# Banded attention in front of two expert layers: the order of q/k loads and x stores on SyncE, and the step in which the next pair is transposed

## The reference, cut to what matters

```python
def _attn_ref(q, k, v, n_global, n_local):          # q, k, v: (4, 8, 768, 64)
    scores = matmul(q, k.T) / sqrt(D)
    keep = is_global | is_local                      # key < 8, or 0 <= row - key < 96
    scores = where(keep, scores + bias, -1e9)        # bias = -slope[head] * distance
    a = exp(scores - max);  a = a / (sum(a) + 1e-9)
    return matmul(a, v)

x = attn.transpose(0, 2, 1, 3).reshape(3072, 512)
x = _moe_ref(x, ...)       # 8 experts, each token to its best one; 512 -> 1024 -> 512
return _moe2_ref(x, ...)   # 8 experts, 384 tokens each, assigned by falling logit
```

## Time and profile before

| | |
|---|---|
| time, median of 3 runs | 1249.87 us (1248.23 to 1251.53) |
| profiled execution: its own time / span | 1250.35 us / 1248.7 us |
| attention, first scores to last product with v | 14.35 to 324.8 us of the span |
| PE busy over the span | 982.6 us (79%) |
| DVE busy over the span | 760.6 us (61%) |
| ACT busy over the span | 411.6 us (33%) |
| queue of SP's transfers | 99.67 MB, 26.7% of 16 engines' span |

### The profile page before, as it was taken

The page is one execution under the profiler, slowest core; times in us unless marked ns, Lnnn a source line. Parts: engine busy times, 40 slices in busy tenths (PEclk is TensorE's granted clock), DMA queues, the critical chain, the costliest instruction groups (busy, mean ns, idle before and its releaser), DMA issues.

```text
span 1248.7 us, 22576 instructions
## 1 busy us (share of the span) xinstructions
PE 982.6 (79%) x6264; PEld 836.7 (67%) x6265; DVE 760.6 (61%) x1994; ACT 411.6 (33%) x885; POOL 193.8 (16%) x242
## 2 busy tenths in 40 slices
PE   7867787878835999999999995122227999999995
PEld 4656666667734788888888884121217889999884
DVE  5656565656675668878786877555564445544441
ACT  3434343434451543442453441000002334433320
POOL 2121111211000111112111111100002122233310
PEclk8888787878976999999999997555556999999998
DMA  8343443434410615343432413000001444455300
GB/s 191 88 98 93 90 97 86 100 82 97 163 68 26 232 35 177 111 157 116 169 119 101 171 70 108 19 1 0 0 0 51 152 168 146 158 184 185 118 26 26
DMA packets 146021, 127.31 MB, mean 102 GB/s; under 512 B 102381, under 2 KB 114669, under 8 KB 145840
## 3 DMA queue, kind: packets, MB, share of 16 engines
q1 hardware_dynamic: 137168, 99.67, 26.7%
q0 software_dynamic: 8800, 27.01, 6.3%
HBM read 107.78 MB, written 20.71 MB: 103 GB/s over the span
## 4 chain that ended last, share of the span: by engine, by line
PE 47%; DVE 15%; issue 6%; DVEq 3%; ACT 1%; ACTq 1%; DMA 0%; POOL 0%; POOLq 0%
PE ps_o L1150 9%; PE ps_s L1127 8%; PE ps_o L1519 7%; PE ps_s L1503 6%; PE ps_pT L1503 5%; DVE product L1348 4%; PE ps_s L1519 4%; PE ps_t L1677 2%; PE ps_pT L1138 1%; PE ps_t L960 1%; DVEq L1351 1%; DVE arena_t L1768 1%; DVE w_split_parts L1339 1%; PE ps_t L1490 1%; PE ps_t L1113 1%
## 5 line engine op out<-in xcount | busy, mean ns | idle before, releaser
L1150 PE MATMUL ps_o<-w_split_parts,hs 128*128 x696 | 170.4, 401 | 9.9 <-ACT hs L1226 9.1
L1127 PE MATMUL ps_s<-w_split_parts,xs 128*128 x696 | 167.9, 397 | 2.3 <-issue 1.4
L1150 PEld LDWEIGHTS ps_o<-w_split_parts,hs 128*128 128x128 f32 x696 | 131.4, 192 | 38.5 <-issue 11.3
L1348 DVE SCALAR_TENSOR_TENSOR product<-y_sb,wg_all 128x512 bf16<-128x512 f32 x232 | 151.0, 689 | 7.2 <-ACT y_sb L1244 2.2
L1127 PEld LDWEIGHTS ps_s<-w_split_parts,xs 128*128 128x128 f32 x696 | 130.1, 190 | 29.6 <-issue 3.4
L638 DVE CUSTOM_DVE_ANT_0 arena_p<-ps_s,arena_b 128x256 f32<-128x256 f32 (+1 forms) x144 | 54.1, 392 | 113.9 <-PE ps_s L442 57.0
L758 ACT ACTIVATE arena_p<-arena_p,min_s 128x256 f32<-128x256 f32 (+1 forms) x192 | 91.8, 484 | 12.0 <-DVE min_s L638 10.6
L1519 PE MATMUL ps_o<-w_split_parts,hs 128*128 128x512 f32 x384 | 94.2, 397 | 0.0
L1339 DVE TENSOR_TENSOR w_split_parts<-raw,w_split_parts 128x1024 f32 (+1 forms) x68 | 78.7, 1221 | 5.7 <-ACT w_split_parts L1237 4.4
L1546 ACT ACTIVATE xs<-ps_t 128x512 fp32r<-128x512 f32 x22 | 13.2, 600 | 206.2 <-PE ps_t L1490 206.1
L1519 PEld LDWEIGHTS ps_o<-w_split_parts,hs 128*128 128x128 f32 x384 | 70.2, 188 | 16.1 <-ACT hs L1553 2.9
(11 more groups left out here) (287 smaller groups left out, 1842.3 us busy)
## 6 DMA issues: line engine op xcount, KB each, us to landing
raw<-in_moe_w SPq DMA_DIRECT2D x32, 2048.0 KB, 9.4
y_rows<-y_sb POOLq DMA_DIRECT2D x31, 256.0 KB, 2.3
kn<-in_k SPq DMA_DIRECT2D x32, 192.0 KB, 3.4
qn<-in_q SPq DMA_DIRECT2D x32, 192.0 KB, 3.5
vn<-in_v SPq DMA_DIRECT2D x32, 192.0 KB, 2.8
x_rows<-arena_x SPq DMA_DIRECT2D x96, 64.0 KB, 1.6
va<-in_v SPq DMA_DIRECT2D x32, 120.0 KB, 2.6
wg_rows<-in_moe_w_gate SPq DMA_DIRECT2D x1, 2048.0 KB, 7.6
```

Source lines behind the costliest of these rows:

```text
L1127: last = nc.tensor.matmul(ps_s[:, f, :], xs[:, a, c * P:(c + 1) * P], weights(par, w, cols), start=(n == 0), stop=(n == len(passes) - 1))
L1150: last = nc.tensor.matmul(ps_o[:, 0, :], hs[:, a, c * P:(c + 1) * P], weights(par, 2 + w, slice(c * DM, (c + 1) * DM)), start=(n == 0), st ...
L1348: nc.vector.scalar_tensor_tensor(product[:, e % 2, :], y_sb[:], 1.0, wg_all[:, e, :], ALU.mult, ALU.mult, accum_out=log_now[:, e:e + 1])
```

## The change

On SP the loads of q and k are pulled one pair ahead: the loads of pair 2 are issued once before the loop, and `pair_io` of pair p then issues the loads of pair p+3 (behind a wait for the transposes of pair p+1), the loads of v of pair p+2 and the stores of pair p. The loads of q and k of a pair thus stand in front of the stores of the pair three before it, where they stood behind them. The `wait_ge` and the numbers of transfers are the same; only the order on SP is another.

The transposes move from steps 4, 6, 8, 10, 0, 2 to 3, 5, 7, 9, 11, 1, and their splits with them from 5, 7, 9, 11, 1, 3 to 4, 6, 8, 10, 0, 2. In the first loop turn pair 1 keeps its steps 0, 1, 2. Since group 1 of the odd pair is now transposed in step 11, its split falls into step 0 of the next loop turn, which the new `splits_of` names. Nothing is added to or taken from the work of any engine.

```diff
         def turns_of(first, last_one):
 
-            turns = {0: (0, 0), 1: (0, 1), 2: (0, 2)} if first else {0: (0, 1), 2: (0, 2)}
+            turns = {0: (0, 0), 1: (0, 1), 2: (0, 2)} if first else {1: (0, 2)}
             if not last_one:
-                turns.update({4: (1, 0), 6: (1, 1), 8: (1, 2), 10: (2, 0)})
+                turns.update({3: (1, 0), 5: (1, 1), 7: (1, 2), 9: (2, 0), 11: (2, 1)})
             return turns
+
+        def splits_of(first, last_one):
+
+            splits = {} if first else {0: (0, 1)}
+            splits.update({s + 1: which for s, which in turns_of(first, last_one).items() if s + 1 < STEPS2})
+            return splits
...
-                    if s - 1 in turns_of(first, last_one):
-                        nth, g = turns_of(first, last_one)[s - 1]
+                    if s in splits_of(first, last_one):
+                        nth, g = splits_of(first, last_one)[s]
                         low_qk(it * 2 + nth + 1, (nth + 1) % 2, g)
...
+            def next_qk(pair, par):
+
+                sp.wait_ge(qk_turned, pair * 3 + 3)
+                load_qk(pair + 2, par)
+
-            def pair_io(b, g, more):
+            def pair_io(b, g, more_qk, more_v):
                 pair, par = b * HP + g, g % 2
-                if more:
-
-                    sp.wait_ge(qk_turned, pair * 3 + 3)
-                    load_qk(pair + 2, par)
+                if more_qk:
+                    next_qk(pair + 1, 1 - par)
+                if more_v:
+
                     sp.wait_ge(valued, pair * 12 + 12 + ATT0)
                     load_v(pair + 2, par)
                 store_x(b, g, par)
 
+            next_qk(0, 0)
             with sp.Fori(0, B - 1) as b:
                 for g in range(HP):
-                    pair_io(b, g, True)
+                    pair_io(b, g, True, True)
             for g in range(HP):
-                pair_io(B - 1, g, g < HP - 2)
+                pair_io(B - 1, g, g < HP - 3, g < HP - 2)
```

## The result

The changed kernel takes 1158.06 us (median of 4 runs, 1156.59 to 1159.09) against 1250.61 us (4 runs) of the kernel before: a ratio of 0.9262, 95% interval 0.9244 to 0.9279, or 92.5 us less. Forecast: 1161 us, 1153 to 1180. The profiled execution has a span of 1157.5 us.

What follows compares the result with a forecast made beforehand. No engine is full; TensorE's wait for late q and the half clock after it set the pace. A pair of 13.06 + 0.5 = 13.6 us against 20.44, times 13, saves 89 us: 1161 us, range 1153 to 1180.

Steps and rivals of the forecast that it cites:

- The stall costs twice, 3.72 us of waiting and 2.55 us of clock: Before group 0 transposes, each pair: TensorE waits 3.72 us for q, then loses 2.55 us at half speed; both go.
- Its rival: Clock still drops from TensorE's idle gaps up to 0.6 us: 2.55 us a pair come back, 1195 us; chance 0.05.
- The spare time of the loads, 7.7 us: On SP, first store to last q landing takes 8.6 us, with 16.3 us until the transposes: 7.7 us to spare.
- The step takes away the wait for q_low: Before the next pair's first scores: transposes one step forward remove TensorE's wait for q_low, 0.57 us a pair.
- VectorE's meeting of split and division costs 0.5 us a pair: Steps 4 and 10: group 0's split meets a division on VectorE; TensorE waits 0.5 us a pair, ends 0.4 and 1.5.
- the old meeting: Steps 1 and 7 before the change: group 1's split met a division on VectorE, costing TensorE 0.53 us.
- TensorE's own pace of 13.06 us: Pair 1, first scores to first scores: 13.96 us, 13.06 at full clock without its VectorE waits of 0.41 and 0.49.
- the two counted waits: TensorE's short waits for VectorE in pair 1, 0.41 and 0.49 us, taken off 13.96 us to get 13.06.
- First loop turn: nothing, or 1 us lost: Steps 2 and 3: transposed groups of pairs 1 and 2 follow at once, the second waiting for the bank; 0 or 1 us.
- The rival on the slower side: Loads still land late, so step 4 also falls behind the wait at half clock: +41 us, 1291 us; chance 0.02.

Runs made afterwards that it cites:

- the SP order alone: Changed kernel with transposes and splits put back in their old steps, only the new load order on SP kept: 1168.02 us, 0.9342 of the kernel before.
- the early division: Changed kernel with VectorE's divisions of steps 4 and 10 moved to steps 3 and 9: 1151.96 us, 0.9218 of the kernel before.
- the step alone: Changed kernel with SP's old order put back, transposes and splits kept in their new steps: 1266.43 us, 1.0126 of the kernel before.

## Why the prediction was right

*The stall costs twice, 3.72 us of waiting and 2.55 us of clock.* Right, and shown one by one: filling the wait gave 31.6 us where 13 x 2.55 = 33 was expected, and with the SP order alone both parts went, at 1168 us for 1169. The rule of the Trainium skill on micro-idles ("TensorE: Matmul & The Clock Gate", "A second HAM failure mode: psum-queue depth-cycling") doesn't come into play here: with gaps of up to 0.6 us in every pair the granted clock stays at 1.00. Its rival was wrong.

*The spare time of the loads, 7.7 us.* It is 6.8 us, nearly 1 us less, in three small parts: the pair is shorter than I took (13.25 here for 13.6), the distance from stores to landing is 8.8 us (146.72 to 155.5) for 8.6, and the transposes stand 2.36 us behind the first store (146.72 to 149.08) for 2.7.

*The step takes away the wait for q_low.* Right; it is off the list with the step and at 8.5 us without it.

*VectorE's meeting of split and division costs 0.5 us a pair.* Mis-sized: 0.35. Moving the division took nearly all of it away, so the mechanism was right. The term was carried over from the old meeting (0.53). That it came out lower because TensorE has more work of its own between is likely, but no run shows it.

*TensorE's own pace of 13.06 us.* Mis-sized too: 13.28 - 0.35 = 12.93, and 12.84 with the early division. Both terms together are 0.3 us a pair, 4 us in all: the attention ended 92.9 us earlier where 89 were forecast, at 231.9 us for 236. The stages behind it were 1.7 us longer in the profile, within their scatter, and took part of this back, so that 1159.1 us stands against 1161.4 for the profiled execution. That the forecast is off by 3 us and not by 4 is this scatter, and no merit of the sum. The 13.06 held small gaps that the two counted waits don't name. One stands in step 1, whose v product is the short one. In the trace of the SP order alone, where TensorE's own pace is still 13.06 (14.16 less 0.57 and 0.53), the transposes of the probabilities start 0.35 us behind the last products of the scores there (164.80 to 165.15 us). In the changed kernel a group of q/k transposes stands in front of these scores, and the distance is 0.21 us (158.63 to 158.84 us), as in other steps. These 0.14 us are the size of the difference; that nothing else adds to it was not tested.

*First loop turn: nothing, or 1 us lost.* Group 0 of pair 2 waited 1.37 us for q in one profile and 0.86 us for the bank in another; but the scores of pair 2 start at 43.09 us, against 42.93 before, so nearly nothing was lost.

*The rival on the slower side* was priced at 1291 us, with its extra step at half clock. As a kernel (the step alone) it takes 1266: the step that came behind the wait cost its full-clock 2.03 us, since the clock cost 2.56 us a pair there and not more than before. I had multiplied the step by 5.67 / 3.12. The place and the sign were right, and the price should have been 13 x 1.46 = 19 us.

## What to carry to other kernels

A transfer queue that waits for engines is a program of its own: a load inherits every wait that stands in front of it, so ask for each load what it is issued behind, and move it in front of the waits that end latest, here by a whole pair (its buffer was free that long). Count an idle stretch of TensorE such as the ones here, of 2.7 us and more, with the slow work behind it, and check a forecast by adding up one period from its parts until it equals the measured one; here 13.06 + 1.10 + 3.72 + 2.55 = 20.43 against 20.44 us gave the forecast its footing. When such a stall is gone, look at the order within a step next: taking one of VectorE's two extra tasks out of step 4 brought its waits from 5.3 to 0.8 us.

## What the runs showed of the hardware

With q and k loaded behind v, every idle stretch of 2.67 us or more (13 of them, up to 3.79 us) was followed by a fall of the clock, if not always at once: the granted clock was 0.69 and 0.50 in the two 4 us windows shown of that kernel. Gaps of up to 0.6 us in every pair left it at 1.00, and so did single waits of 1.37 us (the changed kernel) and 1.65 us in the first loop turn; no wait in the attention lay between 1.65 and 2.67 us. Behind the attention of the changed kernel TensorE pauses for 2.51 us before 234.38 us, and at 236 to 238 us its clock is 0.50. Unused bf16 products in the gap (3.19 us for 14) kept it at 1.00 through the loop and made the kernel 31.6 us faster, with q landing as late as before. Half speed lasted 5.67 us of steady work behind a wait of 3.47 us, and some 6.5 us behind one of 6.13 us. On average over the pairs the clock cost 2.1 us behind waits of 2.96 us, 2.55 us behind waits of 3.72 us and 2.56 us behind waits of 6.38 us.
